# Ordering the two column halves of a wide matrix product by weight tile

## The reference

```python
kv  = einsum('bhsd,bhse->bhde', k, v)            # linear attention
out = einsum('bhsd,bhde->bhse', q, kv)
x   = out / sqrt(mean(out**2, -1) + 1e-6) * g_norm      # then [8, 576, 512]

h = relu(x @ w_in)                               # 512 -> 1024, first gated block
u, v = h[..., :512], h[..., 512:]
v_n = (v - mean(v)) / sqrt(var(v) + 1e-6)
v_s = einsum('ts,bsd->btd', w_spatial, v_n) + b_spatial
x   = (u * v_s) @ w_out                          # 512 -> 512

h = relu(x @ w_in2)                              # 512 -> 1024, second gated block
c = conv over the tokens, 3 taps, one weight per channel
out = (h * sigmoid(c)) @ w_out2                  # 1024 -> 512
```

## Time and the profile before

| | us |
|---|---|
| median of 3 runs | 882.77 (882.76 to 883.62) |
| span of the profiled execution | 881.3 |
| what a run takes beside that span (882.77 - 881.3) | 1.5 |
| TensorE busy in the span | 864.9 |
| mean granted clock of TensorE, as a share of full speed | 0.997 |

### The profile page before, as it was taken

How to read it: one execution, slowest core, us unless ns; L and a number is a source line. 1 busy time by engine, 2 the same in 40 slices (tenths; PEclk the granted TensorE clock), 3 DMA queues, 4 the chain that set the end, 5 groups by cost and what they waited for, 6 DMA issues and landing times.

```text
span 881.3 us, 15264 instructions
## 1 busy us (share of the span) xinstructions
PE 864.9 (98%) x5610; PEld 803.2 (91%) x5610; DVE 502.8 (57%) x1195; ACT 417.2 (47%) x767; POOL 33.0 (4%) x34
## 2 busy tenths in 40 slices
PE   6989999999999999999999999999999999999998
PEld 5869989999899999989999989898998989899996
DVE  3496674665747567474664828447380837438280
ACT  4463444344343444434344837446472737446371
POOL 4130000000000000000005000000000000000000
PEclk9999999999999999999999999999999999999999
DMA  9825614343143442242112011020302011020101
GB/s 265 222 35 131 144 50 110 107 107 93 30 104 94 107 94 55 79 94 95 54 54 79 31 59 44 36 78 1 102 1 77 37 47 54 36 77 0 48 0 60
DMA packets 106701, 65.90 MB, mean 75 GB/s; under 512 B 81490, under 2 KB 89706, under 8 KB 106668
## 3 DMA queue, kind: packets, MB, share of 16 engines
q1 hardware_dynamic: 106628, 65.45, 27.9%
q10 hardware_dynamic: 40, 0.01, 0.0%
HBM read 46.58 MB, written 18.87 MB: 74 GB/s over the span
## 4 chain that ended last, share of the span: by engine, by line
PE 94%; DVE 2%; DMA 2%; SPq 1%; ACT 0%; issue 0%; ACTq 0%
PE ps L366 47%; PE ps L562 22%; PE ps L386 11%; PE ps L323 4%; PE ps L345 4%; PE ps L359 2%; PE ps L480 2%; PE ps L335 2%; DMA kv_raw<-v_dram 1%; DMA work<-moe_w_out_dram 1%; DVE sq_xn L917 0%; SPq L175 0%; PE ps L466 0%; DVE ssq L898 0%; DVE ms L900 0%; DVE x_gated_split L927 0%
## 5 line engine op out<-in xcount | busy, mean ns | idle before, releaser
L366 PEld LDWEIGHTS ps<-x_gated_split,w_product_split 128*128 128x128 f32 x1536 | 204.3, 188 | 0.5
L366 PE MATMUL ps<-x_gated_split,w_product_split 128*128 128x288 f32 x1536 | 204.8, 294 | 0.0
L562 PE MATMUL ps<-w_in_split,v_hg_split 128*128 128x512 f32 x832 | 194.6, 389 | 0.0
L562 PEld LDWEIGHTS ps<-w_in_split,v_hg_split 128*128 128x128 f32 x832 | 155.7, 188 | 32.0
L1079 DVE SCALAR_TENSOR_TENSOR work<-work,const_cols 128x576 f32<-128x576 f32 x64 | 52.4, 819 | 151.2 <-ACT work L830 151.2
L366 PE MATMUL ps<-w_sp_split,v_hg_split 128*128 128x288 f32 x896 | 125.8, 297 | 0.0
L366 PEld LDWEIGHTS ps<-w_sp_split,v_hg_split 128*128 128x128 f32 x896 | 119.8, 188 | 0.0
L366 PE MATMUL ps<-x_gated_split,w_in_split 128*128 128x288 f32 x768 | 105.6, 296 | 0.0
L366 PEld LDWEIGHTS ps<-x_gated_split,w_in_split 128*128 128x128 f32 x768 | 102.4, 188 | 0.1
L386 PE MATMUL ps<-w_in_split,x_gated_split 128*128 128x512 f32 x384 | 92.9, 398 | 0.0
L386 PEld LDWEIGHTS ps<-w_in_split,x_gated_split 128*128 128x128 f32 x384 | 72.1, 191 | 14.8
(11 more groups left out here) (103 smaller groups left out, 907.2 us busy)
## 6 DMA issues: line engine op xcount, KB each, us to landing
gated_scratch<-work SPq DMA_DIRECT2D x32, 288.0 KB, 2.1
q_raw<-gated_scratch SPq DMA_DIRECT2D x8, 1152.0 KB, 5.5
kv_raw<-k_dram SPq DMA_DIRECT2D x32, 256.0 KB, 4.5
kv_raw<-v_dram SPq DMA_DIRECT2D x8, 1024.0 KB, 7.1
q_raw<-q_dram SPq DMA_DIRECT2D x32, 256.0 KB, 4.5
out_dram<-sq_xn SPq DMA_DIRECT2D x32, 256.0 KB, 2.0
work<-moe_w_in_dram SPq DMA_DIRECT2D x3, 1024.0 KB, 8.2
kv_raw<-moe_w_out_dram SPq DMA_DIRECT2D x1, 2048.0 KB, 8.4
```

Source lines behind the costliest of these rows:

```text
L366: last = pe.matmul(pair[bank][:, c, :], st, mo[:, c * HALF:(c + 1) * HALF], start=(n == 0), stop=(n == len(steps) - 1))
L562: last = pe.matmul(PS[:, ROW_BANK[i], :], x, wout2[:, w, f, :], start=(f == 0 and n == 0), stop=(f == FT - 1 and n == len(PASSES) - 1))
```

## The change

The two loops in `wide` change places. Before, all steps ran for the first half of the columns in the first bank, and then all steps again for the second half in the second bank. Now each step runs for the first half and at once for the second half, with the same stationary tile, and the two banks accumulate side by side. The matmuls are the same ones, with the same operands, and within each bank they keep their order. All three callers are affected.

```diff
             def wide(bank, steps):
 
-                for c in (0, 1):
-                    for n, (st, mo) in enumerate(steps):
+                for n, (st, mo) in enumerate(steps):
+                    for c in (0, 1):
                         last = pe.matmul(pair[bank][:, c, :], st, mo[:, c * HALF:(c + 1) * HALF],
                                          start=(n == 0), stop=(n == len(steps) - 1))
                 return last
```

## The result

The changed kernel takes 884.16 us (median of 20 runs, 882.99 to 884.98), the kernel before 882.67 us (median of 20 runs beside it). The ratio is 1.0018, with a 95% interval of 1.0011 to 1.0024: some 1.5 us slower, at the edge of what was called no change. The prediction of 882.8 us was 1.4 us too low. Single runs of one kernel spread over some 2 us (the kernel before from 881.56 to 883.62), so the median of a few runs can be 1 us off.

What follows compares the result with a forecast made beforehand. The prediction took TensorE's distance between matmul starts in line 366 to bound the kernel. Repeats, bank changes and halves each came to 0, so 881.3 us of span plus 1.5 gave 882.8 us, range 879.5 to 888.5 us.

Steps and rivals of the forecast that it cites:

- no change: Whole kernel: time stays within 0.2%, its own range 881.2 to 884.4 us; chance 0.60.
- What bounds the kernel: TensorE, busy 864.9 of 881.3 us; the distance between starts of line 366's 3200 matmuls sets the time.
- Reusing the weights: In `wide`, 1088 added repeats of a stationary tile save nothing, since a weight load takes place either way: 0 us.
- The rival of 13.6 us less: In `wide`, each of 1088 repeated stationary tiles saves its 12.5 ns surplus, giving 869.2 us; chance 0.04.
- Changing the bank: In `wide`, 2944 added PSUM bank changes cost nothing, bounds 0 to 3.3 ns each: 0 us.
- The slower rival: In `wide`, each of 2944 added bank changes costs up to 3.3 ns, 9.7 us, giving 892.5 us; chance 0.21.
- all halves at the dearer rate: In `wide`, every half runs at the dearer rate, giving 885.5 us; counted within the bank-change rival's 0.21.
- The halves side by side: In `wide`, the 1.7 ns between halves belongs to the operand, so interleaving keeps the 132.5 ns mean: 0 us.
- the sign that order mattered: In `in_product`, starts twelve apart at 1.58 us throughout or 1.60 us throughout, rather than all 1.59.
- all to 133.3 (2.7 us more): In `wide`, the dear end: if sequence causes the difference, alternation brings all matmuls to 133.3 ns, 2.7 us more.
- The odd bank or the second half's offset: In `wide`, two possible operand-side sources of the second half's 1.7 ns: its odd bank or its 1152-byte start.
- The 1.5 us around the span: Whole kernel: 1.5 us added to the profiled span of 881.3 us to reach the median run of 882.8 us.

## Why the prediction was nearly right, and where it failed

- **What bounds the kernel**: right. The time moved with the distance between the matmuls of line 366, which accounts for it (some 1.6 us by the rows, 1.5 measured); the first expectation, that the counts and the readers' waits stay, holds.
- **Reusing the weights, 0**: right, as far as the repeats and the bank changes can be told apart. 5610 loads, and with the same columns the two orders take 25.28 us alike. The rival of 13.6 us less is out.
- **Changing the bank, 0**: right, and settled the same way. The slower rival named a price of up to 3.3 ns for a change, and the prediction called the bank change its first suspect; that rival's sign came true and this cause did not. What came true stands in its one sentence on all halves at the dearer rate, which had no chance of its own.
- **The halves side by side, 0**: this is the step that failed. It said "I take the operand", and that the mean of 132.5 ns "is kept in any order". Half of it holds: the dearness comes with the moving operand and not with bank or place. But the prices don't add up by matmul. The ground given, that all three callers have a mean of 132.5 ns, couldn't show that they do, since no row before mixes the two halves in one stretch. `in_product` costs as much as its dear half on average, whether the mixing comes from the new order or from alternating columns in one bank; its starts twelve apart are 1.60 us apart throughout, which the prediction had named as the sign that order mattered. The term was written beside the zero as one end, "all to 133.3 (2.7 us more)", and not taken. `in_product` paid it in full: 1536 / 2 x 1.67 = 1.3 us by the halves, 8 x 0.14 = 1.1 us by the chain. The other two callers paid it in full only in the eighth batch (0.17 us for 208 matmuls). In the seven others `u_product` paid 0.04 us for 96 and `spatial_product` 0.01 us for 112; why so little is open, and what differs there is the attention's matmuls between the calls.
- **The odd bank or the second half's offset**: the prediction left this open. It is the offset, taken against the start of the stationary tile, and of the lengths run only 288 columns had the discount.
- **Against the whole**: the range held the time, and 0.18% lies within what was called the same, though its interval reaches from 0.11 to 0.24%. That "no change" came out is in part luck: the sum had a zero where 1.5 us stood, and had all calls paid in full, the 2.7 us more (885.5 us) would still have been in the range, but 0.3% and no longer "no change".
- **The 1.5 us around the span**: a small misreading that changed nothing in the sum. The 881.3 us are the span of one execution and the 882.77 us the median of three. In the changed kernel's runs, where both numbers stand for the same execution (884.43 and 882.3 us), a run takes 2.1 us beside its span.

Why a difference of placement costs anything, and why mixing takes the discount away, no run here shows. A contention between the reading of the weights and the reading of the moving operand would fit, since only their difference mattered; that is argued, not shown.

## What to carry to other kernels

In a stream that TensorE bounds, measure the distance between starts separately for each operand slice before reordering them: two rates that alternate in long runs didn't average when they were interleaved here. Putting one weight tile's matmuls side by side, or spreading them over two banks, is no gain by itself where every matmul brings its own load. And look where the moving tile starts against the stationary one: a shift of 64 to 192 bytes of some tiles cost this kernel 4 to 9 us without any change to its work.

## What the runs showed of the hardware

- Float32r matmuls of 512 columns, start to start at the full clock, cost 226.7 ns where moving and stationary operand start at the same remainder of 256 bytes, 229.2 ns where the moving one starts 64 bytes further on, and 233.5 ns at 128 and at 192.
- At 288 columns the difference of 0 gives 131.7 ns, 64 gives 132.5, and 128 and 192 give 133.3; mixing 0 and 128 gives 133.2 in the mean of a batch of `in_product`. Parts of 320 and 256 columns, at a difference of 0, have a mean of 133.3 ns.
- Changing the PSUM bank at every matmul and repeating the stationary tile, both at once, made no difference of 0.01 us in 192 matmuls.
- VectorE's subtraction on 576 float32 columns took some 1.8 us in the stretch in which GpSimd worked on its own tiles, and 0.75 us otherwise. That the two engines hindered each other is not shown by a run without GpSimd's work.
